# An attention stage rebuilt: gate columns beside the values, keys pooled in 96 partitions, values added in pieces into their tile

## The reference

```
# attention: B=8, H=8, S=576, D=64, pool=8, so 72 pooled keys per head
k_p = k.reshape(B, H, 72, 8, D).mean(axis=3)
v_p = v.reshape(B, H, 72, 8, D).mean(axis=3)
scores = (q @ k_p.T) / sqrt(D);  scores -= scores.max(-1)
attn = exp(scores);  attn /= attn.sum(-1) + 1e-9
x = (attn @ v_p), heads side by side           # (4608, 512)
# routing: 8 experts, the best two of each token
logits = x @ w_gate
noise_scale = log1p(exp(x @ w_noise))
noisy = logits + noise_scale * noise
# ... top 2, softmax over them, expert MLP 512-1024-512, sum
# then one more MLP 512-2048-512 with h - tanh(h)
```

## Time and profile before

| | us |
|---|---|
| median of three runs (2071.35 to 2075.60) | 2073.27 |
| the profiled execution | 2070.45 |
| its span (first to last instruction) | 2068.7 |
| attention, up to the last normalised head | 311.0 |
| first product of the experts | 359.72 |
| PE, DVE, ACT, POOL busy over the span | 1942.2, 1055.1, 836.8, 562.8 |

### The profile page before, as it was taken

The page is one execution under the profiler, slowest core; times in us unless marked ns, Lnnn a source line. Parts: engine busy times, 40 slices in busy tenths (PEclk is TensorE's granted clock), DMA queues, the critical chain, the costliest instruction groups (busy, mean ns, idle before and its releaser), DMA issues.

```text
span 2068.7 us, 36878 instructions
## 1 busy us (share of the span) xinstructions
PE 1942.2 (94%) x13280; PEld 1744.3 (84%) x13281; DVE 1055.1 (51%) x2002; ACT 836.8 (40%) x1776; POOL 562.8 (27%) x527
## 2 busy tenths in 40 slices
PE   5888882999999999999999996999999999999999
PEld 5677671989899999999998986889999889999888
DVE  6778864313131313132131316766777766777765
ACT  4566562323232323232232324444444444444444
POOL 3354535112121112112212122222222222322222
PEclk9999995999999999999999998999999999999999
DMA  7545323314131313212131312001000001100000
GB/s 210 135 126 147 102 61 108 126 41 138 46 132 51 122 42 115 66 63 105 56 122 53 129 46 97 32 30 61 30 30 30 30 30 51 40 30 30 30 30 21
DMA packets 79077, 152.34 MB, mean 74 GB/s; under 512 B 12768, under 2 KB 37472, under 8 KB 76224
## 3 DMA queue, kind: packets, MB, share of 16 engines
q1 hardware_dynamic: 62720, 108.42, 16.7%
q0 software_dynamic: 16320, 43.45, 6.3%
HBM read 111.51 MB, written 40.33 MB: 73 GB/s over the span
## 4 chain that ended last, share of the span: by engine, by line
PE 86%; DVE 7%; issue 3%; DMA 2%; POOL 1%; ACT 1%; DVEq 0%; SPq 0%; POOLq 0%; ACTq 0%
PE banks L715 13%; PE banks L714 13%; PE banks L713 13%; PE banks L704 12%; PE banks L705 12%; PE banks L706 12%; PE banks L694 3%; PE banks L601 2%; PE banks L620 2%; PE banks L580 1%; PE banks L589 1%; DVE kp L1022 1%; DMA v_raw<-in_v 1%; DVE mx L1033 1%; DMA k_raw<-in_k 1%
## 5 line engine op out<-in xcount | busy, mean ns | idle before, releaser
L704 PE MATMUL banks<-x_hi,w_hi 128*128 128x256 f32 x2304 | 639.3, 277 | 5.1 <-DVE x_lo L1232 4.1
L705 PE MATMUL banks<-x_lo,w_hi 128*128 128x256 f32 x2304 | 638.6, 277 | 0.0
L706 PE MATMUL banks<-x_hi,w_lo 128*128 128x256 f32 x2304 | 638.6, 277 | 0.0
L713 PE MATMUL banks<-w_hi,h_hi 128*128 128x512 f32 x1184 | 467.1, 395 | 3.0 <-DVE h_lo L1256 3.0
L715 PE MATMUL banks<-w_hi,h_lo 128*128 128x512 f32 x1184 | 466.1, 394 | 0.0
L714 PE MATMUL banks<-w_lo,h_hi 128*128 128x512 f32 x1184 | 463.0, 391 | 0.0
L704 PEld LDWEIGHTS banks<-x_hi,w_hi 128*128 128x128 f32 x2304 | 435.1, 189 | 8.1 <-DVE x_lo L1232 4.9
L705 PEld LDWEIGHTS banks<-x_lo,w_hi 128*128 128x128 f32 x2304 | 435.2, 189 | 2.5
L706 PEld LDWEIGHTS banks<-x_hi,w_lo 128*128 128x128 f32 x2304 | 435.0, 189 | 0.0
L542 POOL TENSOR_SCALAR large<-u_sq 128x512 uint8<-128x512 f32 x144 | 222.6, 1546 | 585.5 <-ACT u_sq L971 317.6
L1239 DVE SCALAR_TENSOR_TENSOR h_lo<-banks,h_hi 128x512 fp32r<-128x512 f32 x144 | 99.6, 692 | 379.7 <-ACT h_hi L922 379.7
(11 more groups left out here) (141 smaller groups left out, 2223.7 us busy)
## 6 DMA issues: line engine op xcount, KB each, us to landing
w_raw<-in_moe_w SPq DMA_DIRECT2D x32, 1024.0 KB, 5.0
y<-y_rows SPq DMA_DIRECT2D x18, 1024.0 KB, 5.0
k_raw<-in_k SPq DMA_DIRECT2D x32, 288.0 KB
q_sb<-in_q SPq DMA_DIRECT2D x32, 288.0 KB, 10.5
v_raw<-in_v SPq DMA_DIRECT2D x8, 1152.0 KB
x_rows<-x_sb SPq DMA_DIRECT2D x32, 288.0 KB, 3.6
out_x<-y_sb SPq DMA_DIRECT2D x36, 256.0 KB, 2.1
w_raw<-in_moe_w_in SPq DMA_DIRECT2D x4, 1024.0 KB, 4.9
```

The costliest lines, as they stand in the source:

```text
L704: pe.matmul(part, hi, x_hi[:, c, :], start=(c == 0), stop=False)
L705: pe.matmul(part, hi, x_lo[:, c, :], start=False, stop=False)
L706: mm = pe.matmul(part, lo, x_hi[:, c, :], start=False, stop=(c == NC - 1))
L713: pe.matmul(p_y[m][:, :], hi, w_hi[par][:, o:o + DM], start=(j == 0), stop=False)
```

## The change

- **Gate columns beside the values.** `VW` becomes 81: 64 values, 16 gate columns, one denominator column. Since x is a weighted mean of value rows, x @ w is the same weighted mean of (value rows @ w). So once a batch and half (four heads) the pooled values are transposed (`values_cols`, four transposes), copied by ACT to `vT`, multiplied with a head's 64 rows of `wg` (`gate`, four small products) and copied by ACT into columns 64 to 79 of `vp`. `normalise` then makes two products: `x_sb` as before, and `lgp` (16 columns of each head); `part0` adds the eight heads' `lgp` in three steps. `x_cols`, `xT_a`, the old `gate`, `gate_rows`, `gl` and ACT's copies for them go. The 1e-9 of the denominator comes from rows 64 to 127 of `vp` and a `pT` set to 1.0 at the start, so the `den` instruction goes.
- **Two output banks.** `p_o` becomes two single banks by turns, and `values(u)` waits for `normalised` one head further back.
- **Keys.** `k_raw` holds half a batch in 96 partitions, one contiguous run each; `pool_keys` handles four heads in three additions (768, 384 and 384 elements a partition), the last one written twice, instead of four reductions and a copy.
- **Values.** POOL adds two heads at a time and the last addition goes straight into `vp`; `v_stage` and DVE's copy go. It waits for `pv_done` of the batch before. The 12 scatters are issued in two sixes between.
- **Order.** Routing parts 0 to 5 of the batch before now stand in slots 1, 2, 3, 4, 6 and 7 of the next; the keys in slots 0 and 5. SP's order of loads is new, and q, k and v of the first batch come in other pieces.

The diff, cut to what the steps need:

```diff
-        X_ORDER = ["x0", "x1", "k1", "x2", "g0", "x3", "g1", "gt", "x4", "x5", "x6", "k0", "x7", "cs"]
+        X_ORDER = [("vb0", 0), ("k1", 0), ("va1", 0), ("vb1", 0), ("cs", -1), ("k0", 1), ("va0", 1)]
...
@@ SP
-            sp.dma_start(k_raw[:, 0, :, :], k_v[:, 0:2, :]).then_inc(k_in[0], 16)
+            load_k(0, 0)
             load_q(0, 0)
-            for p in range(1, PAIRS):
-                load_k(0, p)
-                load_q(0, p)
-            load_v(0)
+            load_v(0, 0)
+            load_k(0, 1)
+            load_q(0, 1)
+            load_v(0, 1)
+            load_q(0, 2)
+            load_q(0, 3)
...
@@ POOL
+            def add_v(b, p):
+
+                if p % 2 == 0:
+                    pool.wait_ge(v_in[p // 2], (b + 1) * 16)
+                v = v_raw[:, 2 * p:2 * p + 2, :, :]
                 for i, j in enumerate((4, 2)):
+                    pool.tensor_tensor(v[:, :, 0:j, :], v[:, :, 0:j, :], v[:, :, j:2 * j, :], ALU.add).then_inc(v_added, 1)
+                    pool.wait_ge(v_added, b * 2 * PAIRS + (2 * p + i + 1))
+
+            def pool_v(b, p):
+
                 if not is_first(b):
+                    pool.wait_ge(pv_done, (b - 1) * H + (2 * p + 2))
+                v = v_raw[:, 2 * p:2 * p + 2, :, :]
+                pool.tensor_tensor(vp[0:KEYS, 2 * p:2 * p + 2, 0:D], v[:, :, 0, :], v[:, :, 1, :], ALU.add
+                                   ).then_inc(vp_ready, 1)
...
+            def body(b, back=True):
+                if not is_first(b):
+                    pool_v(b, 3)
                 if not is_last(b):
+                    add_v(b + 1, 0)
+                    add_v(b + 1, 1)
+                if back:
+                    scatter(b - 2, (0,))
+                if not is_last(b):
+                    pool_v(b + 1, 0)
+                    pool_v(b + 1, 1)
+                    add_v(b + 1, 2)
+                    add_v(b + 1, 3)
+                if back:
+                    scatter(b - 2, (1,))
+                if not is_last(b):
+                    pool_v(b + 1, 2)
...
@@ PE
-                wait(pe, normed, b * H + u)
-                if u == 0:
-                    pe.wait_ge(vp_ready, b + 1)
+                wait(pe, normed, b * H + (u - 1))
+                if u % PAIRS == 0:
+                    pe.wait_ge(x_bank, x_use(b, f"vb{u // PAIRS}") + 1)
...
+            def values_cols(b, part, use):
+
+                pe.wait_ge(vp_ready, b * PAIRS + (2 * part + 2))
                 pe.wait_ge(x_bank, use)
+                settle(pe)
+                for a in range(PAIRS):
+                    mm = pe.transpose(p_x[0:D, a * KEYS:(a + 1) * KEYS], vp[0:KEYS, part * PAIRS + a, 0:D], ident[0:KEYS, 0:KEYS])
+                mm.then_inc(v_tr, 1)
+
+            def gate(b, part, use):
 
                 pe.wait_ge(x_bank, use)
                 if is_first(b):
+                    pe.wait_ge(loads0, 3 * 16)
+                for a in range(PAIRS):
+                    mm = pe.matmul(p_x[0:KEYS, a * GW:(a + 1) * GW], vT[:, a * KEYS:(a + 1) * KEYS],
+                                   wg[:, part * PAIRS + a, :], start=True, stop=True)
+                mm.then_inc(vg_done, 1)
...
+                    if s == 0 and not first:
+                        gate(b, 0, x_use(b, "vb0"))
                     if s == 1:
                         keys(b, 1, x_use(b, "k1"))
...
+                    if s == 3:
+                        values_cols(b, 1, x_use(b, "va1"))
+                    if s == 4:
+                        gate(b, 1, x_use(b, "vb1"))
+                    if s == 5 and not first:
+                        positions(b - 1, x_use(b, "cs", -1))
+                    if s == 6 and not is_last(b):
+                        keys(b + 1, 0, x_use(b, "k0", 1))
+                    if s == 7 and not is_last(b):
+                        values_cols(b + 1, 0, x_use(b, "va0", 1))
...
@@ ACT
-            def gate_rows(b):
-                act.wait_ge(gt_done, b + 1)
-                wait(act, m_ready, b)
-                act.activation(lg[:, :, :].rearrange("p t e -> p (t e)"), p_x[0:TP, 0:TT * 2 * E], ACT.Copy
-                               ).then_inc(x_bank, 1)
+            def values_cols(b, part):
+                act.wait_ge(v_tr, b * 2 + (part + 1))
+                act.activation(vT[:, :], p_x[0:D, 0:PAIRS * KEYS], ACT.Copy).then_inc(x_bank, 1)
...
@@ DVE
+            def pool_keys(b, part):
+
+                dve.wait_ge(k_in[part], b * 16 + 16)
+                half = CD // 2
+                for i in range(2):
+                    k2 = k_raw[:, part, :, :]
+                    dve.tensor_tensor(k2[:, :, 0:half], k2[:, :, 0:half], k2[:, :, half:2 * half], ALU.add).then_inc(k_halved, 1)
+                    dve.wait_ge(k_halved, b * 4 + (part * 2 + i + 1))
+                    half //= 2
+                wait(dve, k_tr, b * 2 + (part - 1))
+                both = [k_raw[:, part, :, i * D:(i + 1) * D].unsqueeze(2).to_broadcast([KP, KC, 2, D]) for i in range(2)]
+                dve.tensor_tensor(kp[:, part, :, :, :], both[0], both[1], ALU.add).then_inc(k_pooled, 1)
...
-                dve.tensor_scalar(den[:, :, :], o4[:, :, :, D], POOL * 1e-9, None, ALU.add).then_inc(denned, 1)
-                dve.wait_ge(denned, b * 2 * H + (2 * u + 1))
-                dve.reciprocal(rden[:, :, :], den[:, :, :]).then_inc(denned, 1)
-                dve.wait_ge(denned, b * 2 * H + (2 * u + 2))
+                dve.reciprocal(rden[u % 2][:, :], o4[:, :, D + GW]).then_inc(denned, 1)
+                dve.wait_ge(denned, b * H + (u + 1))
                 wait(dve, x_out[u // 2], b * 16)
...
+                dve.tensor_tensor(lgp[:, u, :, :], o4[:, :, D:D + GW], rden[u % 2][:, :].unsqueeze(2).to_broadcast([TP, TT, GW]), ALU.mult
                                   ).then_inc(normed, 1)
-
-            def copy_v(b):
-                dve.wait_ge(v_pooled, b + 1)
-                dve.tensor_copy(vp[0:KEYS, :, 0:D], v_stage[:, :, :]).then_inc(vp_ready, 1)
...
+                dve.wait_ge(normed, b * H + H)
+                for n in (4, 2):
+                    step(0, b, dve.tensor_tensor(lgp[:, 0:n, :, :], lgp[:, 0:n, :, :], lgp[:, n:2 * n, :, :], ALU.add))
+                step(0, b, dve.tensor_tensor(lg[:, :, :], lgp[:, 0, :, :], lgp[:, 1, :, :], ALU.add))
...
+                    if s == 0:
+                        pool_keys(b, 1)
+                    if s == 5 and not is_last(b):
+                        pool_keys(b + 1, 0)
+                    if not is_first(b):
+                        if s == 1:
+                            part0(b - 1)
+                        if s == 2:
+                            part1(b - 1)
+                        if s == 3:
+                            part2(b - 1)
+                        if s == 4:
+                            part3(b - 1)
+                        if s == 6:
+                            part4(b - 1)
+                        if s == 7:
+                            part5(b - 1)
```

More of the change, by code:

```diff
@@ L614, in gate @@
-            def gate(b, half, use):
+                settle(pe)
[3 more added lines that the diff above has]
+            def gate(b, part, use):
                 pe.wait_ge(x_bank, use)
                 if is_first(b):
-                    pe.wait_ge(loads0, 9 * 16)
-                for c in range(NC):
-                    mm = pe.matmul(p_x[0:2 * E, 0:HT], wg[:, c, :], xT_a[:, c, half * HT:(half + 1) * HT], start=(c == 0), stop=(c == NC - 1))
-                mm.then_inc(g_done, 1)
@@ L865, in body @@
                         probs_cols(*at)
-                    if s == H - 1 and not is_last(b):
-                        keys(b + 1, 0)
-                    if s == 4 and not is_first(b):
-                        gate_rows(b - 1)
                     if s < H - 1:
@@ L889, in _ @@
             probs_cols(last, 7)
-            for s in range(4):
-                x_cols(*x_part(B, s))
-                if s >= 2:
-                    gate(last, s - 2)
-            gate_rows(last)
             exps_of_noise(last)
```

301 lines of the change are left out of this document (117 added, 184 removed).

## The result

The changed kernel takes 2054.63 us (median of four runs, 2054.45 to 2059.50) beside 2072.31 for the kernel before on the same chip: a ratio of 0.9919, 95% interval 0.9899 to 0.9938. It is faster, by some 17 us, under 1%, and the forecast said 64: 2054.6 lies above the range of 1980 to 2041. The profiled span is 2052.8 us.

A forecast was written before the change was run, and what follows sets the result against it. DVE's order was to bound attention's batches, 30.1 us instead of 37.40. Start 43.8 + 6 x 30.1 + 29.9 for the last batch + tail 12.0 = 266.3 instead of 330.2, so 63.9 less: 2009 us, range 1980 to 2041.

The forecast's parts named there:

- the bank wait: Slot 6: PE's next key transposes wait for the shared bank until DVE's part 4; costs about 1.3 us.
- The step on POOL: POOL's additions and scatters take 24 us of a 30.1 us batch; some 3 us of slack, so it does not bound.
- The rival "no gain": Waits for vp only move to POOL, batches stay at 36 to 38 us; total 2050 to 2075; chance 0.07.
- The step on the lock: DVE's two-SBUF-input additions beside POOL's, some in slots 1 and 5, lose little: 0.9 us a batch.
- my bound of 5.8: Upper limit, in us a batch, for DVE additions with two SBUF inputs running beside POOL's; the lower was nothing.
- the rival "lock": DVE and POOL additions exclude each other: batch 32 to 34.7 us, total 2022 to 2041; chance 0.22.
- PE: PE needs 21 us a batch, with 0.19 us a slot saved by 81 columns, and no longer bounds.
- The clock's 0.35 us: Allowance a batch for PE's clock dropping during its new waits, taken from between nothing and 2 us.
- The slots: Eight slots a batch, counted between row maximum ends, limited by DVE's parts or values' latency: 28.85 us in sum.
- its two additions: 0.9 us for DVE beside POOL and 0.35 for the clock, 1.25 together, taking 28.85 to 30.1 us a batch.
- The start: Batch 0: first values at 23.4 us, 6.2 earlier than before; batch 1 starts at 43.8.
- The tail: After the last normalisation: last twelve scatters start 12.0 us later instead of 19.2, held by POOL; gain 7.2 us.

The follow-up runs named there:

- experiment 6: Changed kernel with a separate slot_i per batch: alone 2056.57 us; with the fold as one reduction and part 4 early 2042.49; with all experiment 5 edits 2025.20.
- experiment 5: Changed kernel with lgp folded by one reduction, part 4 in slot 5, DVE's key additions in slot 6, PE's key transposes in slot 7: 2052.04 us.
- the last kernel: Changed kernel with all experiment 5 edits and a separate slot_i per batch, so DVE does not wait for scatters: 2025.20 us, ratio 0.9784.
- part 4 early: Changed kernel with DVE's routing part 4 issued in slot 5 ahead of the key additions instead of in slot 6: 2061.70 us, ratio 0.9947.

## Why the prediction was wrong

Two steps failed, and either alone keeps a batch at about 37 us. With the wait for the scatters away, the lock and the bank wait behind it hold it at 37.3 (the first of the kernels of experiment 6); with the lock and bank edits alone, the scatters hold it at 37.9 in batch 4 (experiment 5). So mending one step would not have saved the forecast.

**The step on POOL** is "then waits again for slot 1: some 3 us of slack. It does not bound." The work was about right (forecast 3.9 us for the four halvings of two pairs, 4.2 measured in experiments 5 and 6). What was left out is who waits for POOL. The change splits the twelve scatters into six and six and puts the second six behind the values of head 3; DVE's part 5, two slots later, waits until they have landed. My own numbers could have shown it: 0.4 + 3.9 + 7.3 = 11.6 us from the start of slot 5, and then the landing, where my table left 3.9 + 3.65 + 2 = 9.6 to part 5. Measured it is 15.1. In the kernel before the twelve stood in one run at the start of a batch and DVE never waited there, so no row of before priced the wait; the line of code did. The rival "no gain" had the result, 2050 to 2075, and nearly the reason ("POOL has 24 us of work in a fixed order with waits on PE"), and I gave it 0.07 on the strength of that slack. Its own mechanism, the waits for `vp` moving to POOL, was not it: POOL idles for 76 us in front of `vp` between 60 and 330 us, waiting for PE's values, and PE waits for no write of `vp` by POOL between 60 and 270 us.

**The step on the lock** is "so I take little, 0.9". It was priced at 0.9 us a batch from the earlier trace rows and measured 4.2: (1.69 + 1.21 + 0.71) - (0.94 + 0.26 + 0.20) = 2.2 in slot 1 and (2.67 + 1.40) - (1.53 + 0.56) = 2.0 in slot 5. It is inside my bound of 5.8. Together with the bank wait and the clock (below) it left the batch at 37.3 us with the scatters' wait away, above the 34.7 of the rival "lock". The earlier trace rows was the wrong row to be nearest to, and the earlier trace rows, with the copies at 2.65 and 1.76, the better one. The POOL instruction of rows 9 has one input, those of rows 2 and of this kernel have two; whether that is the reason was not tested. The page of the Trainium skill that I had set against the earlier trace rows (SBUF — State Buffer, "Who interferes with whom") is what this kernel's additions follow: `TENSOR_TENSOR` with both inputs in SBUF is stretched beside POOL, the reduction is not (0.95), products of PSUM and SBUF are not (L1051 0.55 throughout). It also counts copies and `tensor_scalar` among the forms that can contend, by a mode of their own; the 0.89 us of L1127 agrees, and so do the copies of the earlier trace rows. These have one input, so the prediction was not right to count the key copy under the rule on two inputs.

**PE.** Its work was forecast at 21 us, and is 24 in the last kernel. The 0.19 us a slot for 81 columns instead of 100 are not there: `probs` starts 1.03 us behind `values` with 81 columns (178.25 to 179.28) and 1.03 with 100 (186.53 to 187.56). Slot 6's wait on the bank was forecast as a gap of 2 us that costs 1.3, and measured 3.6; the stretched key additions stand ahead of part 4. The clock's 0.35 us was far too little in the changed kernel (values in slot 7 2.21 instead of 1.20, scores 1.65 instead of 0.95, two of each at the lower level or part of it: an estimate of 3 us of PE's time), and about right where the period is 30.8 (1.00). What lets the clock fall stays open.

**The slots** held within 0.5 us, but for slot 7. With both limits gone they are 3.61, 3.39, 4.28, 3.75, 3.17, 3.77, 3.82, 4.97, beside 3.5, 2.9, 4.1, 3.6, 3.15, 3.9, 3.65, 4.05: a sum of 30.76 for 28.85, or 30.1 with its two additions. That the sums come so close is in part luck: in that kernel part 4, the keys and PE's key transposes stand in other slots than in the forecast, and PE's work is 3 us more.

**The start**: values at 22.39 (forecast 23.4), but batch 1 at 47.1, not 43.8: batch 0's slots 2 and 7 took 5.9 and 6.8 us. (By the same count batch 1 began at 50.0 before, not at the 53.2 of the prediction; the sum does not use it.)

**The tail**: the last twelve scatters start 13.7 us behind the last normalisation, forecast 12.0. DVE meets the same wait there:

```profile
314.06 0.17 DVE L1150 COPY row_id<-row_all 96x12 int32<-96x12 int32 x1 [2.48 <-DMA slot_row<-row_id,slot_i]
...
315.16 0.92 POOL L477 DMA_INDIRECT slot_row<-row_id,slot_i  x1 [2.33 <-DVEq L1153]
```

**The rest of the gap.** The best kernel is still 16 us above 2009. Its first expert product is at 315.6, mine was at 295.8 (the stage behind and the chip's own kernel before are 1 to 2 us shorter each): its batch 1 starts at 50.4 instead of 43.8, and batches 1 to 3 took 34.4, 32.0 and 35.7 us, only 4 to 6 took 30.5 to 30.8. Why the early ones are longer was not followed.

## What to carry to other kernels

When a change splits or moves an engine's work, list who waits for the end of each piece, a buffer's reuse among them, and add the chain up from its last input to that waiter; slack of the engine as a whole says nothing on it. A wait of under a microsecond that is there in every period can mark a second limit of nearly the same length: edits that shorten only one of the two measure as little or nothing, so try them together before giving one up. What lies ahead of both still pays alone. And price an exclusion between two engines from a row with the same kinds of operands on both.

## What the runs showed of the hardware that I had not expected

- A DVE `TENSOR_SCALAR` with one input of six elements a partition took 0.89 us beside POOL's additions (part 4 early), 0.16 elsewhere; DVE's 768-element reduction took 0.95 in all eight batches, beside them or not.
- DVE went on 1.3 to 1.6 us after the last of six scatters was issued in the changed kernel, and 4.0 to 4.5 us after it in batches 2 to 5 of experiment 5, where the DMA engines' busy share in that time was some 0.6 instead of under 0.3.
- On some chips the kernel before takes 4% longer (2157 us for 2071), and the traces kept there show DVE and ACT waiting for PE's products twice a batch, mostly 3 to 5 us and up to 8, with nothing in the profile that ends the wait.
- PE without a gap still fell to the lower clock: during 7.45 us of 16-column products the granted clock went from 1.00 to 0.50, and the scores behind took 1.65 us. In the fastest kernel waits of 2.5 us before the key transposes left it at the upper level (clock 1.00 over batch 4).
